# First rounding step of the cosine argument on GpSimd in the first tiles, and an earlier read of h

## The reference

```
w   = softmax(weight, axis=-1)              # 8 heads x 7 taps
x1  = causal convolution of x with the 7 taps of its head
h   = x1 @ moe_w_in                         # 192 -> 2048
x2  = (h * cos(h)) @ moe_w_out              # 2048 -> 192
out = (relu(x2 @ moe2_w_in) ** 2) @ moe2_w_out
```

## Time and profile before

| | us |
|---|---|
| median of 3 runs | 2252.88 |
| execution with the profile | 2253.41 |
| its span | 2251.1 |
| TensorE busy | 2239.1 (99%) |
| VectorE busy | 1774.6 (79%) |
| ScalarE busy | 1734.8 (77%) |
| GpSimd busy | 0.2 (0%) |

### The profile page before, as it was taken

The page is one execution under the profiler, slowest core; times in us unless marked ns, Lnnn a source line. Parts: engine busy times, 40 slices in busy tenths (PEclk is TensorE's granted clock), DMA queues, the critical chain, the costliest instruction groups (busy, mean ns, idle before and its releaser), DMA issues.

```text
span 2251.1 us, 46857 instructions
## 1 busy us (share of the span) xinstructions
PE 2239.1 (99%) x19526; PEld 2213.3 (98%) x19526; DVE 1774.6 (79%) x1813; ACT 1734.8 (77%) x1844; POOL 0.2 (0%) x4
## 2 busy tenths in 40 slices
PE   8999999999999999999999999999999999999999
PEld 7899999999999999999999999999999999999998
DVE  8887788777787777887778877778877788777773
ACT  6677777777877777777778777787777787777876
POOL 0000000000000000000000000000000000000000
PEclk9999999999999999999999999999999999999999
DMA  4000000000000000000000000000000000000000
GB/s 127 27 15 15 9 14 12 10 14 7 14 14 7 14 9 13 14 7 14 14 7 14 14 7 14 7 14 14 7 14 14 7 14 14 7 14 7 7 8 15
DMA packets 13456, 33.26 MB, mean 15 GB/s; under 512 B 1905, under 2 KB 1905, under 8 KB 13169
## 3 DMA queue, kind: packets, MB, share of 16 engines
q1 hardware_dynamic: 13280, 32.81, 4.9%
q10 hardware_dynamic: 144, 0.00, 0.0%
HBM read 20.22 MB, written 12.58 MB: 15 GB/s over the span
## 4 chain that ended last, share of the span: by engine, by line
PE 97%; DVE 2%; ACT 1%; issue 0%; DMA 0%
PE h L346 10%; PE h L350 10%; PE h L348 10%; PE h L352 10%; PE y_A L402 5%; PE y_A L396 5%; PE y_A L400 5%; PE y_A L398 5%; PE y_A L404 5%; PE h L355 5%; PE y_B L400 5%; PE y_B L398 5%; PE y_B L396 5%; PE y_B L404 5%; PE y_B L402 5%; DVE conv L712 0%
## 5 line engine op out<-in xcount | busy, mean ns | idle before, releaser
L698 DVE TENSOR_TENSOR g_lo<-g,g_hi 128x1024 fp32r<-128x1024 f32 x512 | 625.2, 1221 | 272.0 <-ACT g_hi L545 271.1
L545 ACT ACTIVATE g_hi<-g 128x1024 fp32r<-128x1024 f32 x512 | 538.3, 1052 | 44.1 <-DVE g L694 43.4
L537 ACT ACTIVATE w<-w,quarter 128x1024 f32<-128x1024 f32 x256 | 295.5, 1154 | 304.6 <-DVE w L688 304.6
L396 PE MATMUL y_A<-g_hi,dn_lo_A 64*128 64x512 f32 x1024 | 396.9, 388 | 0.1
L402 PE MATMUL y_A<-g_hi,dn_side_A 64*128 64x512 f32 x1024 | 396.3, 387 | 0.0
L398 PE MATMUL y_A<-g_hi,dn_hi_A 64*128 64x512 f32 x1024 | 396.0, 387 | 0.0
L400 PE MATMUL y_A<-g_lo,dn_hi_A 64*128 64x512 f32 x1024 | 395.8, 387 | 0.0
L404 PE MATMUL y_A<-g_lo,dn_side_A 64*128 64x512 f32 x1024 | 395.8, 387 | 0.0
L348 PE MATMUL h<-x_hi_A,up_lo_A 64*128 64x512 f32 x1024 | 394.5, 387 | 0.0
L352 PE MATMUL h<-x_hi_A,up_hi_A 64*128 64x512 f32 x1024 | 394.5, 386 | 0.0
L350 PE MATMUL h<-x_lo_A,up_hi_A 64*128 64x512 f32 x1024 | 394.4, 386 | 0.0
(11 more groups left out here) (122 smaller groups left out, 6180.0 us busy)
## 6 DMA issues: line engine op xcount, KB each, us to landing
xt<-x SPq DMA_DIRECT2D x32, 393.0 KB, 3.1
out<-late SPq DMA_DIRECT2D x32, 256.0 KB, 2.0
out<-late SPq DMA_DIRECT2D x32, 128.0 KB, 2.3
late<-w_out SPq DMA_DIRECT2D x2, 1536.0 KB, 9.5
stage_in_side<-w_in SPq DMA_DIRECT2D x2, 512.0 KB, 4.2
stage_in_side<-w_in SPq DMA_DIRECT2D x4, 256.0 KB, 5.3
w<-w_in SPq DMA_DIRECT2D x1, 768.0 KB, 7.1
stage_in_side<-w_in SPq DMA_DIRECT2D x2, 384.0 KB, 9.1
```

What stands on the lines that cost most here:

```text
L396: mm = pe.matmul(sums[:, 0, :], dn_lo[kind][rows, c, :], hi, start=a, stop=False)
L545: act.activation(g_hi[:, s % RING, :, :], g[:, s % RING, :, :], ACT.Copy).then_inc(hi_made[kind], 1)
L698: dve.tensor_tensor(g_lo[:, r, :, :], g[:, r, :, :], g_hi[:, r, :, :].bitcast(F32), ALU.subtract).then_inc(lo_made[kind], 1)
```

## The change

In turn 0 the pairs A1 to A7, and in turn 1 the pairs A1 and A2, get line 686 (the `whole` step) from GpSimd instead of VectorE. GpSimd waits for `taken`, and for `g_made` of the pair two back, since that pair has the same buffer of `w`. VectorE waits for the new semaphore `pool_whole` and goes on with line 688. The first tap of the convolution for tile two is made by GpSimd too. In turn 0 ScalarE now copies `h` of the slot's pair before it makes the sine of the pair before; the order of the other engines stays. In the loop and in the last turns nothing is moved.

```diff
+POOL_PAIRS, POOL_TAP = {0: (1, 2, 3, 4, 5, 6, 7), 1: (1, 2)}, (0, 0)
...
@@ scalar, body @@
                     back, last, q, runs = turn.earlier(s, 1)
+
+                    h_first = turn.peeled and turn.i == 0 and kind == "A"
+                    if h_first:
+                        read_h(turn, s, kind, p)
                     if last == "A" and runs:
                         turned_cosine(turn, q, back)
...
-                    if turn.runs(kind):
+                    if turn.runs(kind) and not h_first:
                         read_h(turn, s, kind, p)
@@ vector, fraction @@
-                dve.wait_ge(taken["A"], turn.count("A", p))
-                dve.tensor_scalar(v, u, 0.25, ROUND, ALU.add, ALU.add).then_inc(whole, 1)
-                dve.wait_ge(whole, turn.count("A", p))
+                if on_pool(turn, p):
+                    dve.wait_ge(pool_whole, pooled(turn, p))
+                else:
+                    dve.wait_ge(taken["A"], turn.count("A", p))
+                    dve.tensor_scalar(v, u, 0.25, ROUND, ALU.add, ALU.add).then_inc(whole, 1)
+                    dve.wait_ge(whole, turn.count("A", p) - pooled(turn, p))
...
-                        if turn.runs("C") and s == taps_at[k]:
+                        if turn.runs("C") and s == taps_at[k] and not (turn.peeled and (turn.i, k) == POOL_TAP):
...
+        @block.gpsimd
+        def _(pool):
+            def whole_turns(turn, r, p):
+                if turn.i == 0 and p < WB:
+                    pool.wait_ge(wi_lo, 4)
+                if turn.count("A", p) > WB:
+                    pool.wait_ge(g_made, turn.count("A", p) - WB)
+                pool.wait_ge(taken["A"], turn.count("A", p))
+                pool.tensor_scalar(w[:, p % WB, :, :], g[:, r, :, :], 0.25, ROUND, ALU.add, ALU.add)\
+                    .then_inc(pool_whole, 1)
+            def first_tap(turn):
+                pool.wait_ge(x_loaded, (turn.i + 2) * 16)
+                pool.wait_ge(x1_hi, 3 * (turn.i + 1))
+                pool.wait_ge(x1_made, turn.i + 1)
+                pool.tensor_scalar(conv_parts, parts[:, :, 0:HALF_TOK], taps[:, 0:1], None, ALU.mult)\
+                    .then_inc(tap_done, 1)
```

More of the change, by code:

```diff
@@ L60, with on_pool, pooled @@
 FIRST_PART = 2 * PAIR * P
+POOL_PAIRS, POOL_TAP = {0: (1, 2, 3, 4, 5, 6, 7), 1: (1, 2)}, (0, 0)
+def on_pool(turn, p):
+    return turn.peeled and p in POOL_PAIRS.get(turn.i, ())
+def pooled(turn, p):
+    if not turn.peeled:
+        return sum(map(len, POOL_PAIRS.values()))
+    return sum(i < turn.i or i == turn.i and q <= p for i, pairs in POOL_PAIRS.items() for q in pairs)
 TWO_PI = 2.0 * math.pi
@@ L227, in tile_program @@
         whole = sem("whole")
+        pool_whole = sem("pool_whole")
         frac = sem("frac")
@@ L784, in _ @@
             turns(dve, body)
+        @block.gpsimd
[14 more added lines that the diff above has]
+                    .then_inc(tap_done, 1)
+            for i in POOL_PAIRS:
+                turn = Turn(i, TILES)
+                if i == POOL_TAP[0]:
+                    first_tap(turn)
+                for s, (kind, p) in enumerate(turn.slots()):
+                    if kind == "A" and on_pool(turn, p):
+                        whole_turns(turn, s % RING, p)
 def kernel(x, weight, moe_w_in, moe_w_out, moe2_w_in, moe2_w_out):
```

## The result

The changed kernel takes 2261.42 us (median of 7 runs, 2260.14 to 2263.28) against 2253.2 us for the kernel before on the same chips (7 runs, 2252.74 to 2253.6): 8.2 us slower, a ratio of 1.0037 with a 95% interval of 1.0027 to 1.0047. The profiled execution has a span of 2260.0 us, 8.9 over the 2251.1 of before; it was the slowest of the seven (2263.28 us), whose spans go from 2258.3 to 2261.4. The forecast was 2249.8 us with a range to 2256.8; it was wrong in sign.

A forecast was written before the change was run, and what follows sets the result against it. VectorE was taken to set the time at the start of tile one, TensorE being full later. Terms -1.64 - 1.71 + 0.31 = -3.04 us from 2252.88 gave 2249.8 us (chance 0.52), range 2248.7 to 2256.8.

The forecast's parts named there:

- GpSimd's instructions: Duration of a rounding step on GpSimd: taken as 1.2 us, bounded by 0.69 and 2.29 from other engines' rows.
- A second term: VectorE's multiplications and lines 688 in tile one: durations stay at 1.22 us beside GpSimd, no cost in the sum.
- rival 1: GpSimd holds VectorE up in tile one, each step costing its whole duration: 2254.5 us at 1.2, 2262 at 2.29; chance 0.30.
- Tile two: A1's step on GpSimd ends later than VectorE's, so the start at 82.00 comes 0.31 us later.
- A0's `g_lo`: Ahead of TensorE's start at 31.41: tap and A1's rounding step leave VectorE's queue, start 1.64 us earlier.
- That is why both parts are needed: Start at 31.41: with VectorE relieved alone, A2's read behind the sine would still hold TensorE.
- The starts of A6 and A7: At 42.66 and 48.00: VectorE's round falls to 4.52 us, waits for reads go, 1.71 us gained together.
- Hidden in tile one?: Tile one: line 688 comes 4.5 us after the read, 3 for A1, so GpSimd's 1.2 or 2.29 us is hidden.
- The tap: First tap on GpSimd starts at 15.8 to 16.76 us, is needed at some 30 us, and costs nothing.
- The clock: After the idle time ahead of the start at 31.41, the clock falls as before, at the same cost, about 1.8 us.
- Rival 2: Clock stays up after the start at 31.41; 0.5 us of the gain remains, 2249.3 us; chance 0.08.
- Rival 3: GpSimd's rounding steps cost VectorE what they free; only tap 0.9 and early read 0.2 us gain, 2251.8 us; chance 0.10.

The follow-up runs named there:

- aside_ts: The kernel before, plus nine GpSimd tensor_scalar instructions from a weight tensor into its own buffer, for which nobody waits: 2259.32 us, ratio 1.0028.
- tap: The kernel before with only the first tap of tile two's convolution moved to GpSimd: 2252.44 us, ratio 0.9997.
- window: The kernel before, plus four measuring phases ahead of VectorE's first work, with GpSimd instructions beside small VectorE ones: 2268.35 us, one run.
- tile_one: The changed kernel, but tile two's A1 and A2 keep their rounding step on VectorE: 2256.8 us, ratio 1.0018.
- aside_set: As aside_ts, with nine memsets of 128x1024 into GpSimd's own buffer in place of the tensor_scalar: 2254.01 us, ratio 1.0004.
- read_tap: The kernel before with the early read of h in tile one and the first tap on GpSimd, all rounding steps on VectorE: 2252.20 us, ratio 0.9995.
- read: The kernel before with only the early read of h in tile one, nothing on GpSimd: 2252.95 us, ratio 0.9998.
- spread_dve: As spread, with the first tap on VectorE too, so GpSimd does nothing: 2251.93 us, ratio 0.9995.
- spread: As read_tap, with the six other taps of tile one moved to later slots: 2250.81 us, ratio 0.9989.

## Why the prediction was wrong

**The step that failed** is "GpSimd's instructions", where the duration was "bounded from rows: not under the 0.69 us ... and not over 2.29 us" and set to 1.2. It is 3.63 us alone and 3.68 to 5.10 in the kernel. The rows chosen as neighbours were of VectorE and ScalarE; none was of GpSimd, so they bounded nothing. The upper end of the range, 2256.8, hung on the same number.

**A second term was put at nothing**: the forecast has VectorE's durations "stay at 1.22 us", and a price for the two engines at one memory stands in rival 1 alone. Nine instructions in aside_ts for which nobody waits, eight of them with a hold, cost 6.2 us. The duration by itself does not explain the miss. With 3.68 us, tile two gives +2.8, and at A1 the step would end at about 27.1 (its read ends at 23.29), where line 688 was to start at 26.13, so that about 1.0 of the 1.64 us is lost. The prediction's sum is then -1.64 + 1.0 - 1.71 + 2.8, about +0.4 us, an estimate from these rows; 8.2 were measured. The rest is the holds, what follows from them on GpSimd, and the clock.

**Tile two**: "come 0.31 us later". The form of the sum was right, the release at 77.64 and the step's end deciding; with 3.68 us it gives 77.64 + 0.06 + 3.68 - 78.59 = 2.8 us, and 7.03 - 4.12 = 2.91 us were measured (4.12 us late is A7's down product, which starts at 70.76 in place of 66.64). The 0.06 us for the release stood on no row of GpSimd; the changed kernel took 0.15, from the end of the read at 81.79 to 81.94. On this came a fall of the clock. Removing the two steps gave back 4.6 us.

**A0's `g_lo`**: "The `g_lo` then ends at 29.63". The 1.64 us did leave VectorE's queue; 3.24 us came in, as read above: 1.56 us of waiting, since GpSimd's first step lasted 5.10 us, and 2 x 0.84 us of delay. "That is why both parts are needed" did not hold either: tap, without the early read, had this start 0.99 us sooner, since the sine of A1 and the read behind it moved with VectorE.

**The starts of A6 and A7**: the waits for reads went, as forecast. VectorE's round was said to be 4.52 us. It has lost the rounding step (0.72) and got a delay of 0.84 or 0.68 us, and every other time 0.6 us of waiting; from the line 710 at 28.58 to that at 62.92 six rounds take 34.34 us, 5.72 each, where the same six took 5.43 before (27.77 to 60.34; the first has a weight split in it). So the down product of A4 now waits, 1.9 us, and behind it the clock falls.

**Hidden in tile one?** "1.2 is hidden, and 2.29 would be too" was right as to kind: of the 3.7 us the waits show 1.56 us at A1 and 0.62 at each second pair. **The tap**: it started at 18.05 us, behind the load of x, and not at 15.8 as predicted, and still cost nothing: the rows of VectorE beside it are no longer than before, and the next tap came at 33.98 us.

**Rival 1** had the right side, and the wrong price. It charged the whole duration for each step; at 3.7 us that is 2252.88 + 1.6 + 7 x 2.5 = 2272 us, against 2261.4. The hold on an instruction with two inputs is 0.85 us, as window shows. The Trainium skill's rule ("SBUF — State Buffer", section "Who interferes with whom") is borne out in that two-input instructions of VectorE meet GpSimd's reads (1.79 us for 1.01) and not its writes alone (the taps beside the memsets keep 1.01), and that a fast one-input form meets a memset (1.38 for 0.69). Its sentence that the other is blocked for the whole instruction is not: 27 instructions with two inputs ran in the 2.64 us that were left of GpSimd's 3.63, and 19 with one input between their two holds. The estimate of 0.88 us from the Trainium skill's "GPSIMD Engine Reference" (section 3.1) fits that hold, 0.85 us, and not the duration.

**The clock**: "as before, at the same cost". It fell three times, behind the idle time that was there and the two new ones of 1.95 and 3.58 us. The length of an idle time does not settle it: there was no fall behind 2.02 us in tile_one and 1.87 us in tap, and one behind 1.40 us in aside_set. What decides is open. **Rival 2**, that the clock stays up, did not come, as the first idle time grew; in tap, where it shrank to 1.87 us, it did, and as the rival had it little remained: the next start there, 36.34, waits 1.30 us for a read. **Rival 3** put tap and read alone at 1.1 us under before; read_tap, which is that, came out 1.05 us under by the medians, with an interval that holds none.

How the 8.2 us divide, by medians: read and tap -1.05, tile one's seven steps +4.6 (tile_one less read_tap), tile two's two steps +4.6 (changed kernel less tile_one). The last two hold to a microsecond or so, since tile_one's runs lie in two groups. How tile one's 4.6 us divide between waiting and delay is not settled to better than the rows above: neither was taken away without the other.

## What to carry to other kernels

Before work moves to an engine that the trace shows idle, have a row of that engine for that operation; rows of other engines give no bound, and one run with the instruction alone settles it. Then count twice: the duration where somebody waits, and the delay that each instruction causes on its neighbour even if nobody waits. If the neighbour is full, and gives up 0.72 us but is held 0.85 us, nothing can come of it. A single slow instruction still pays where it has time: the first tap takes 2.5 us on GpSimd and brought 0.7 to 1.1 us by the medians (tap; read_tap less read; spread_dve less spread). A gain of about the same size, 0.9 to 1.2 us, lay in moving the other taps on VectorE itself to where it has room.

## What the runs showed of the hardware

- GpSimd's two-operation tensor_scalar on fp32 128x1024 takes 3.63 us alone, with one operation 2.78, a memset of that size 0.95; VectorE's two-operation form takes 0.69.
- While GpSimd is at that tensor_scalar, a VectorE instruction with two inputs is held once, at its start, for 0.85 us by 1024 elements and 0.42 us by 512. The small one-input form is held at the start (0.88 us) and again until GpSimd's end, and by a memset until its end. The one-input tap (1.00 us) beside the first instruction of aside_ts was not held, nor was the rounding step of VectorE at 46.19 us (0.68), which lies between the start and the end of GpSimd's.
- GpSimd in turn waits for the end of VectorE's instruction with two inputs. Its steps of 5.10, 4.12 and 4.54 us began inside such rows, and each ended 3.5 us behind the end of that row (25.04, 29.81 and 37.25 us).
- In the kernel read the idle time before the first joined slot grew from 2.79 to 4.29 us, since A3's up product was done sooner, and the mean clock from 20 to 40 us was 0.83 in place of 0.91, another 1.6 us. Work that only comes sooner can cost clock, as it did here.
